# Moving the splits of w_out and the edges of the expert loops in an attention, expert and gated-MLP kernel

## The reference

```python
def _moe_ref(x, modality_id, w_gate, modality_bias, w1, w2):      # N=2304, D=512, E=8, F=1024
    logits = x @ w_gate + modality_bias[modality_id]
    e_idx = np.argmax(logits, axis=1)
    ...
    for e in range(E):
        mask = e_idx == e
        if not mask.any():
            continue
        h = np.maximum(x[mask] @ w1[e], 0.0)
        out[mask] = gate_w[mask, None] * (h @ w2[e])

def _moe2_ref(x, w_in, w_out):                                    # 2304x512, 512x2048, 2048x512
    h = x @ w_in
    sp = np.where(h > 20.0, h, np.log1p(np.exp(np.minimum(h, 20.0))))
    g = h * np.tanh(sp)
    return (g @ w_out).astype(np.float32)
```

## Time and profile before

| what | us |
|---|---|
| median of 3 runs | 940.85 |
| lowest, highest | 934.74, 943.63 |
| the profiled execution's own time | 939.59 |
| its span | 938.0 |
| TensorE busy | 905.8 (97%) |
| VectorE busy | 653.3 (70%) |
| ScalarE busy | 513.6 (55%) |
| GpSimd busy | 477.5 (51%) |
| mean granted TensorE clock | 0.989 |

### The profile page before, as it was taken

One profiled execution on the slowest core, in us unless ns is written; L12 is line 12 of the kernel. 1 busy time (PEld: TensorE's weight loads), 2 busy tenths in 40 slices (PEclk: granted clock), 3 DMA queues, 4 the chain that ended last, 5 costly groups with the idle time before them and its releaser, 6 DMA issues.

```text
span 938.0 us, 19257 instructions
## 1 busy us (share of the span) xinstructions
PE 905.8 (97%) x7004; PEld 764.0 (81%) x7005; DVE 653.3 (70%) x1190; ACT 513.6 (55%) x1098; POOL 477.5 (51%) x557
## 2 busy tenths in 40 slices
PE   6999999999999999999889899999999999999997
PEld 4777777777778888888778788898889899889985
DVE  5898999989856111111233998888788788788793
ACT  4898888999871212121324655555455455555552
POOL 4222225556522490001300786786777777776885
PEclk9999999999999999999989899999999999999999
DMA  3122235433134940202081100001001000000000
GB/s 130 54 81 74 74 133 204 187 110 101 34 103 165 341 156 1 95 7 88 0 295 38 66 1 27 19 23 34 29 7 34 35 1 1 35 1 1 34 1 34
DMA packets 21448, 66.95 MB, mean 71 GB/s; under 512 B 3184, under 2 KB 3184, under 8 KB 20592
## 3 DMA queue, kind: packets, MB, share of 16 engines
q1 hardware_dynamic: 14432, 40.19, 12.9%
q0 software_dynamic: 4192, 20.00, 5.6%
q10 hardware_dynamic: 2736, 5.60, 1.9%
HBM read 47.22 MB, written 18.57 MB: 70 GB/s over the span
## 4 chain that ended last, share of the span: by engine, by line
PE 63%; DVE 4%; issue 2%; DMA 1%; ACT 1%; SPq 0%; POOL 0%; ACTq 0%; POOLq 0%; DVEq 0%
PE psum L1503 7%; PE psum L1504 6%; PE psum L1505 6%; PE psum L1493 6%; PE psum L1495 6%; PE psum L1494 6%; PE psum L1162 4%; PE psum L1163 4%; PE psum L1164 4%; PE psum L1177 4%; PE psum L1178 4%; PE psum L1176 4%; DVE rr L1632 2%; PE psum L1148 1%; PE psum L1477 1%
## 5 line engine op out<-in xcount | busy, mean ns | idle before, releaser
L1632 DVE RECIPROCAL rr<-rr 128x384 f32<-128x384 f32 x96 | 244.0, 2542 | 9.2 <-ACT rr L1569 9.2
L1246 DVE SCALAR_TENSOR_TENSOR hT_lo<-psum,hT_hi 128x512 fp32r<-128x512 f32 (+1 forms) x40 | 26.6, 664 | 157.2 <-ACT hT_hi L1223 157.0
L1493 PE MATMUL psum<-x2T_hi,w_in_hi 128*128 128x384 f32 x384 | 131.6, 343 | 1.1 <-DVE x2T_lo L1644 0.8
L1441 POOL TENSOR_TENSOR uu<-uu,ex 128x384 f32<-128x384 f32 x96 | 97.5, 1015 | 67.3 <-ACT uu L1561 67.2
L1495 PE MATMUL psum<-x2T_hi,w_in_lo 128*128 128x384 f32 x384 | 130.1, 339 | 0.0
L1494 PE MATMUL psum<-x2T_lo,w_in_hi 128*128 128x384 f32 x384 | 129.6, 337 | 0.0
L727 DVE TENSOR_SCALAR_CACHE_REDUCE ssb<-psum,tauk 128x576 f32<-128x576 f32 x144 | 112.6, 815 | 23.6 <-PE psum L426 20.4
L574 ACT ACTIVATE prob<-ssb,smin 128x576 f32<-128x576 f32 x144 | 113.0, 787 | 26.9 <-DVE ssb L727 26.2
L1503 PE MATMUL psum<-w_hi,g_hi 128*128 128x512 f32 x288 | 115.6, 401 | 2.6 <-DVE gg L1640 2.6
L1504 PE MATMUL psum<-w_lo,g_hi 128*128 128x512 f32 x288 | 115.1, 400 | 0.0
L1505 PE MATMUL psum<-w_hi,g_lo 128*128 128x512 f32 x288 | 115.0, 399 | 0.0
(11 more groups left out here) (215 smaller groups left out, 2070.4 us busy)
## 6 DMA issues: line engine op xcount, KB each, us to landing
qk<-in_qk_dram SPq DMA_DIRECT2D x15, 640.0 KB, 4.2
vsb<-in_v_dram SPq DMA_DIRECT2D x16, 512.0 KB, 3.7
xrow<-xs ACTq DMA_DIRECT2D x15, 288.0 KB, 3.2
ys<-ysb SPq DMA_DIRECT2D x4, 1028.0 KB, 5.8
wa<-in_wa_dram SPq DMA_DIRECT2D x8, 512.0 KB, 5.8
w_in_raw<-in_w_in_dram POOLq DMA_DIRECT2D x4, 1024.0 KB, 13.9
wb<-in_wb_dram SPq DMA_DIRECT2D x8, 512.0 KB, 14.0
yrow<-ys SPq DMA_DIRECT2D x4, 771.0 KB, 4.6
```

What stands on the lines that cost most here:

```text
L1493: pe.matmul(bank_of(n), w_in_hi[:, k, cols], xT_hi[w][:, k], start=(k == 0), stop=False)
L1632: dve.reciprocal(rr[:, n % 4], rr[:, n % 4]).then_inc(r_done, 1)
```

## The change

Four edits, which hang together:

1. The border between two tiles' code in the programs of ScalarE and VectorE moves: a tile now begins with columns 2 and 3 of its own x (x_hi, x_lo), the gate copies and evacuate_y, and ends with columns 0 and 1 of the next x (AHEAD_X = 2). Inside the lead's loop the order of work stays as it was. At an outer loop's start the four pieces of w1 are split between columns 1 and 2.
2. Behind the last tile ScalarE copies and VectorE subtracts pieces 0 to 2 of w_out's first half. The gate copies and the last evacuate_y come behind the three copies. Columns 2 and 3 of the x that follows the last tile, which nothing uses, are left out. Piece 3 stays in the MLP phase, at step 0 (copy) and step 1 (subtraction).
3. w_out's second half is split by GpSimd, between its load of the first chunk's rows and its load of the second chunk's, piece k when the last tile has used piece k of w2 for the last time. ScalarE's and VectorE's four steps for it in the MLP phase go.
4. Waits that this needs: ScalarE's x_high(1, 0) waits for all of the second half (its target lies over wb), and the first x_high and x_low wait for the two columns.

```diff
+AHEAD_X = 2
...
-        with pool.Fori(1, ranks) as r:
+        def split_second(r, first):
+            pool.wait_ge(t["w2_next"], 16 * WP * r)
             for k in range(WP):
                 cols = slice(k * PIECE, (k + 1) * PIECE)
...
                 if k < WP - 1:
                     pool.wait_ge(w2_used, first * (WP - 1) + k)
                 else:
...
+        with pool.Fori(1, ranks) as r:
+            first, end = span(pool, r)
+            split_second(r, first)
+        pool.wait_ge(y_stored, 16 * first_rows + 16)
...
+        load_rows(0)
+        split_second(ranks, tiles)
+        pool.wait_ge(y_stored, 16 * tiles + 16)
...
+        load_rows(1)
...
         def tile(i, wide):                      # ScalarE
+            for k in range(AHEAD_X, KT):
+                x_hi(i, k, wide)
+            move_gates(i)
+            gate_of(i, wide)
             evacuate_y(i, LEAD_W)
             for f in range(FT1):
                 h_hi(i, f, wide)
                 if f == 2:
                     load_x(act, i + 1, wide)
-            for k in range(KT):
+            for k in range(AHEAD_X):
                 x_hi(i + 1, k, wide)
-            move_gates(i)
-            gate_of(i + 1, wide)
...
+        act.wait_ge(t["w1_next"], 16 * WP * ranks)
+        act.wait_ge(up_done, FT1 * tiles)
+        for k in range(WP - 1):
+            cols = slice(k * PIECE, (k + 1) * PIECE)
+            act.copy(w1_hi[:, cols], wa[:, cols]).then_inc(w1_hi_done, 1)
+        move_gates(tiles)
+        gate_of(tiles, OTHER_W)
         evacuate_y(tiles, OTHER_W)
...
         def tile(i, wide):                      # VectorE
+            for k in range(AHEAD_X, KT):
+                x_lo(i, k, wide)
             for f in range(FT1):
                 h_lo(i, f, wide)
-            for k in range(KT):
+            for k in range(AHEAD_X):
                 x_lo(i + 1, k, wide)
...
+        for k in range(WP - 1):
+            w1_low(ranks, k)
...
         def x_high(c, k, w):                    # MLP phase
             act.wait_ge(turned, c * KT + k + 1)
+            if c == 1 and k == 0:
+                act.wait_ge(w2_ready, WP * ranks + WP)
+            if c == 0 and k == 0:
+                act.wait_ge(x_out, KT * tiles + AHEAD_X)
...
         def later_w1_high(c, n):
-            if n < 2:
-                w1_high(2 + n)
+            if n == 0:
+                w1_high(WP - 1)
...
         def w1_steps(c, n):
-            for k in ((0, 1), (2,), (3,))[n] if n < 3 else ():
-                w1_low(k)
+            if n == 1:
+                w1_low(WP - 1)
```

More of the change, by code:

```diff
@@ L1074, in gpsimd @@
         lead_tiles = lead_end(pool)
-        with pool.Fori(1, ranks) as r:
+        def split_second(r, first):
+            pool.wait_ge(t["w2_next"], 16 * WP * r)
             for k in range(WP):
                 cols = slice(k * PIECE, (k + 1) * PIECE)
-                if k == 0:
-                    first, end = span(pool, r)
-                    pool.wait_ge(t["w2_next"], 16 * WP * r)
                 if k < WP - 1:
@@ L1300, in vector, with w1_low @@
         tiles, ranks = counts(dve)
+        def w1_low(r, k):
+            cols = slice(k * PIECE, (k + 1) * PIECE)
+            dve.wait_ge(w1_hi_done, WP * r + (k + 1))
+            dve.tensor_tensor(w1_lo[:, cols], wa[:, cols], w1_hi[:, cols].bitcast(F32),
+                              ALU.subtract).then_inc(w1_ready, 1)
         def tile(i, wide):
+            for k in range(AHEAD_X, KT):
+                x_lo(i, k, wide)
             for f in range(FT1):
                 h_lo(i, f, wide)
-            for k in range(KT):
+            for k in range(AHEAD_X):
                 x_lo(i + 1, k, wide)
@@ L1407, in run @@
                 op(chunk, turn_steps(chunk).index(f), chunk % 2)
-        return run
-    def first_steps(op):
-        def run(c, n):
-            if 4 <= n < 4 + 2 * WP and n % 2 == 0:
-                op(n // 2 - 2)
         return run
@@ L1585, in later_w1_high @@
         def later_w1_high(c, n):
-            if n < 2:
-                w1_high(2 + n)
-        def w_high(k):
-            cols = slice(k * PIECE, (k + 1) * PIECE)
-            act.copy(w2_hi[:, cols], wb[:, cols]).then_inc(w2_hi_done, 1)
+            if n == 0:
+                w1_high(WP - 1)
         def out_copy(columns):
@@ L1677, in vector @@
         read_ids(0, 0)
-        pipeline(dve, [(0, clamp), (0, w1_steps), (1, invert), (2, product), (0, next_ids), (0, next_chunk(x_low)),
-                       (0, first_steps(w_low))], DEPTH)
+        pipeline(dve, [(0, clamp), (0, w1_steps), (1, invert), (2, product), (0, next_ids), (0, next_chunk(x_low))], DEPTH)
     return {"sync": sync, "gpsimd": gpsimd, "tensor": tensor, "scalar": scalar, "vector": vector}
```

42 lines of the change are left out of this document (12 added, 30 removed).

## The result

The changed kernel takes 925.42 us (median of four runs, 924.42 to 927.02) where the kernel before took 940.31 beside it: ratio 0.9863, 95% interval 0.9829 to 0.9897. By that ratio it is faster by 1.4%; the two medians themselves are 1.6% apart. The profiled execution took 924.42 us, 15.2 less than that of before, with a span of 922.8.

What follows compares the result with a forecast made beforehand. TensorE, busy 97%, was the bound; its waits and low clock gave a 17.9 us ceiling. 2.8 (outer loop) plus 5.8 (MLP phase) took 8.6 off 939.59, 931.0; with 1.3 for the median, 932.2 us, range 927 to 939 (8 in 10).

Steps and rivals of the forecast that it cites:

- The outer loop's start: Where w1 is split: TensorE's loss falls from 7.5 to 4.7 us, a gain of 2.8 us.
- it needs 1.41 us for branches and table loads: At the outer loop's start, ScalarE's gap ahead of its first w1 copy stays 1.41 us, so copying starts at 462.47.
- The walk of the turns: Outer loop: VectorE's piece 2, GpSimd's copy, then piece 3 until 469.2; TensorE waits 3.0 us.
- Other turn of the port: Rival, outer loop: GpSimd's copy precedes VectorE's piece 2, -0.7 us there, 935.7 us; chance 0.26 together with two clock falls.
- The border: Between last down and MLP's up(0): everything comes 1.05 us later, TensorE's wait grows from 0.80 to 1.85 us.
- The first steps, waits: MLP's start: TensorE waits 1.5 us at down(0), where it waited 2.6; reciprocal(0) comes 1 to 2 us later.
- The clock in the MLP: MLP's first steps: slow-clock loss taken as 1.2 us, between bounds of 0 and 2.8.
- every single wait of 2.3 us or more in the rows was followed by a slow stretch: Clock rule read from the profile before; such stretches cost 1.6 to 2.8 us, 1.7 taken at the outer loop.
- Steps 4 to 15: MLP phase: without VectorE's four splits, waits of 0.35 and 2.3 us and a 1.6 us slow stretch go: 4.2 us.
- The attention phase: From the start to tile 0's first up matmul: no gain, 0 us.
- GpSimd late: Rival, border and MLP's start: GpSimd's fourth split ends after 516.05 and delays u(0); 944.5 us if 14 late; chance 0.04.
- clock stays up: Rival, outer loop and MLP phase: no slow clock at either place, 11.5 us gained, 929.3 us; chance 0.20.

Runs made afterwards that it cites:

- ahead4: Changed kernel with all four x copies of the next tile made at a tile's end again (AHEAD_X = 4): 935.56 us, ratio 0.9965 to the kernel before.
- before_again: The kernel before, unchanged, run and profiled once more: 938.83 us, ratio 0.9998.
- no_gpsimd_split: Changed kernel without edit 3, w_out's second half split by ScalarE and VectorE in the MLP phase again: 930.59 us, ratio 0.9937 to the kernel before.
- w1_before_w2: Changed kernel, but at the outer loop GpSimd's fourth w2 piece waits for VectorE's four w1 pieces: 926.22 us, ratio 0.9876 to the kernel before.
- mend_two: As mend_last, but at the border GpSimd's third w_out piece also waits for VectorE's three pieces: 929.02 us, ratio 0.9889 to the kernel before.
- pool_double: Changed kernel with GpSimd's subtraction of the fourth w_out piece at the border done twice: 928.24 us, ratio 0.9903 to the kernel before.
- x2_before_third: As mend_last, but at the border VectorE makes x2T_lo ahead of its third w1_lo piece: 925.61 us, ratio 0.9861 to the kernel before.
- mend_last: Changed kernel, but GpSimd's fourth piece waits for VectorE's w1 pieces, four at the outer loop, three at the border: 926.33 us, ratio 0.9848 to the kernel before.
- after_again: The changed kernel, unchanged, run and profiled once more: 926.24 us, ratio 0.9865 to the kernel before.
- no_first_half: Changed kernel without edit 2, pieces 0 to 2 of w_out's first half split in the MLP phase again: 927.05 us, ratio 0.9896 to the kernel before.
- mend_last_again: mend_last, unchanged, run and profiled once more: 923.76 us, ratio 0.9848 to the kernel before.

## Why the prediction fell short

The direction and the places were right, and the mechanisms at both held in the main (the order of the port's turns, VectorE's splits as the limit of the steps 4 to 15); the size was 8.6 where the profiles differ by 15.2. By the steps of the prediction:

- **The outer loop's start, 2.8 predicted, 4.2 measured.** The failing step is "it needs 1.41 us for branches and table loads". That gap stood, in before, behind two short gate copies; here it was 0.36 us. The length of the instruction just ahead does not explain it, since ahead4 has 0.97 behind an equally long one. Counted from the first instruction behind ScalarE's last wait, the copy of w1 began after 1.93 us in after (457.31 to 459.24), after 2.05 in ahead4 (466.02 to 468.07) and after 2.89 in before (462.73 to 465.62), with the gate copies in between. So the branches and loads seem to run beside instructions that were already handed over. This fits the three places; no run varied it by itself. The walk of the turns behind it was right in its order and came 0.8 us too late at its end (piece 3 at 469.2; 466.19 measured, 468.4 on before's scale). The wait was 1.92 instead of 3.0. The slow stretch, taken at 1.7, cost 1.6: the twelve matmuls from 466.71 to 470.47 took 3.76 us, where 0.177 each makes 2.12.
- **Other turn of the port, -0.7.** It did not come: GpSimd's copy started at 463.91, some 0.9 us after VectorE had begun on piece 2 (460.72 and two pieces of 1.14), where I had counted on 0.3.
- **The border, -1.05 predicted, -0.55 measured.** The wait was 1.35 instead of 1.85. The 0.29 us that I put ahead of the copies for the loops' ends didn't show: the first followed its x_hi at once (498.61, against 497.88 + 0.86 less the overlap). The last evacuation started 0.03 us behind the last matmul's start, and 0.45 ahead of it before, so it moved by 0.48, not by 1.05.
- **The first steps, waits.** Down(0) waited 1.13 us; 1.5 was taken. Against the last down reciprocal(0) came 0.3 us later than before (511.83 against 501.91, and 517.91 against 508.31), where the prediction had 1 to 2.
- **The clock in the MLP, 1.2 taken, 0 measured**, in both profiles of after. This is the largest mis-sized term, before the wait at the outer loop (1.1 us). With the 0.37 us of the wait this is 1.6 of the 2.0 that were missing in C to D; 0.3 more lie in the eight ups, which took 17.03 us in that profile of before and 16.71 in before_again. I had read "every single wait of 2.3 us or more in the rows was followed by a slow stretch" as the price of a shorter wait too; the runs show no such rule, see below.
- **Steps 4 to 15, 4.2 predicted, 4.6 measured.** Right: no wait at up(12), none at chunk 1's turns. With edits 1 and 2 in place edit 3 is worth 6.4 there, as no_gpsimd_split showed.
- **The attention phase, 0 predicted, 2.2 measured**, 1.4 the second time. Its code is the same in both kernels, and in fourteen profiles of it A lay anywhere from 274.20 to 281.76 us. w1_before_w2 and mend_two, which differ only in waits of GpSimd far behind A, were 4.7 us apart. No edit is shown to have caused any of it. Where the differences arise is shown below.
- **GpSimd late (0.04).** No step waited for the fourth piece. The rival's limit was real, though: 2.4 us later costs nothing (pool_double), mend_two and x2_before_third lie beyond, and each waited 1.2 us more at down(0) than after; mend_two had a slow clock too.

**Where the attention phase differed.** With TensorE's matmuls followed one by one through the fourteen profiles, the differences against after arise at four places. By 20 us before, ahead4 and pool_double were 3 us behind, both profiles of mend_last 2.1 us, and after_again, no_first_half and x2_before_third 0.9 to 1.4 us ahead. Between 132 and 146 us up to 1.0 us was gained. Between 249 and 266 us before_again, after_again, mend_last and mend_two lost 2.4 to 2.5 us, 1.5 to 1.6 of it in one wait of TensorE for ScalarE. Just ahead of A ahead4, mend_last_again, mend_two and x2_before_third lost 2.5 to 2.9 us, where TensorE waited 2.4 to 3.0 us for the rows of tile 0's x (1.2 to 1.6 in the other profiles) and the clock was low behind that. One of each (after_again, mend_last_again):

```profile
257.74 0.47 PE L516 MATMUL psum<-wx,otsb 128*64 128x144 f32 x4 [1.56 <-ACT x L612]
...
274.45 1.94 PE L1156 MATMUL psum<-ident,xrow 128*128 128x128 f32 x8 [2.75 <-DMA xrow<-xs]
```

Of before, after and mend_last the two profiles each lay within 0.5 us of each other at A, but by different delays: before was 3 us late by 20 us, before_again lost its 2.5 us at 249 to 266. So that agreement was chance, and the two later delays do not belong to a kernel's code (mend_last's came at one of the places, mend_last_again's at the other). What sets off each delay was not settled.

Without the attention phase, 939.59 - 13.0 is 926.6, and 1.3 more as the prediction counted 927.9: inside the range, at its edge. But it took 13.0 us (12.3 the second time) where the sum had 8.6, so the size was off also without that phase. The rival "clock stays up", 11.5 us, was nearest in number, and in part by luck: it was right for the MLP phase, but at the outer loop the clock did fall, and the 4.2 us there came from a wait that was 1.1 us shorter than any of the rivals had it.

## What to carry to other kernels

Where a gap is put down to branches and loads of registers, ask how much work the engine had been handed since its last wait: the same loads left 0.36, 0.97 and 1.41 us bare at three places. When two engines exclude each other by whole instructions, a stage that is made earlier may slide under a neighbour whose work hangs on a load and didn't move; walk the next stage too before counting a gain. And cut both profiles at the same instructions and subtract stretch by stretch: here 2 us of "gain" lay ahead of everything that the change touches. Two profiles that agree at one instruction can have come there by different delays, so compare them at several.
